# The last chunk's mix: one VectorE pass a tile, each tile on its own semaphore

## The reference, cut to what matters

```python
top2_w = np.exp(top2_l)
top2_w /= top2_w.sum(-1, keepdims=True) + 1e-09
out = np.zeros((N, D), dtype=np.float32)        # N = 2304 tokens, D = 512
for e in range(E):
    for k in range(2):
        mask = top2[:, k] == e
        h = np.maximum(x[mask] @ w1[e], 0.0)
        out[mask] += top2_w[mask, k, None] * (h @ w2[e])
```

## Time and profile before

| what | value |
|---|---|
| median of 3 runs | 1107.4 us (1107.07 to 1108.57) |
| the profiled execution's own time | 1106.87 us |
| its span, first to last instruction | 1105.0 us |
| granted TensorE clock, mean | 0.994 |
| PE busy | 1076.4 us (97%) |
| DVE / ACT / POOL busy | 52% / 29% / 36% |

### The profile page before, as it was taken

One profiled execution on the slowest core, in us unless ns is written; L12 is line 12 of the kernel. 1 busy time (PEld: TensorE's weight loads), 2 busy tenths in 40 slices (PEclk: granted clock), 3 DMA queues, 4 the chain that ended last, 5 costly groups with the idle time before them and its releaser, 6 DMA issues.

```text
span 1105.0 us, 20155 instructions
## 1 busy us (share of the span) xinstructions
PE 1076.4 (97%) x6113; PEld 939.6 (85%) x6114; DVE 575.4 (52%) x1209; ACT 324.3 (29%) x713; POOL 398.7 (36%) x370
## 2 busy tenths in 40 slices
PE   8999999999999999999999999999999999999994
PEld 7878999999998999999987788888888888888883
DVE  6776335254353353353447765565565565565461
ACT  7996123232331432432352102030303020200341
POOL 3557993022022022020185306070706051431485
PEclk9999999999999999999999999999999999999998
DMA  7975527013013012010084526271625253422675
GB/s 215 274 242 192 172 86 276 1 58 115 1 58 116 1 62 92 1 58 1 28 249 159 139 61 186 43 204 38 196 51 170 65 148 92 117 73 61 171 229 187
DMA packets 167356, 129.40 MB, mean 117 GB/s; under 512 B 96720, under 2 KB 128864, under 8 KB 167296
## 3 DMA queue, kind: packets, MB, share of 16 engines
q1 hardware_dynamic: 145440, 71.20, 22.9%
q10 hardware_dynamic: 16032, 38.47, 10.5%
q0 software_dynamic: 5824, 18.95, 5.1%
HBM read 85.87 MB, written 42.73 MB: 116 GB/s over the span
## 4 chain that ended last, share of the span: by engine, by line
PE 87%; POOL 3%; issue 3%; DMA 2%; ACT 2%; DVE 1%; another core or an unknown queue 0%; SPq 0%; POOLq 0%; ACTq 0%; DVEq 0%
PE bank L793 26%; PE bank L957 19%; PE bank L973 18%; PE bank L825 13%; PE bank L986 3%; PE bank L739 2%; PE bank L766 1%; POOL token_rows_a L680 1%; PE bank L749 1%; PE bank L733 1%; DMA token_rows_b<-expert_rows,slots_u 1%; PE bank L861 1%; ACT p_sb L1108 1%; POOL token_rows_a L693 1%; PE bank L872 1%
## 5 line engine op out<-in xcount | busy, mean ns | idle before, releaser
L793 PE MATMUL bank<-x_parts,mlp_weights 128*128 128x384 f32 x1704 | 312.0, 337 | 0.4 <-issue 0.3
L793 PEld LDWEIGHTS bank<-x_parts,mlp_weights 128*128 128x128 f32 x1704 | 296.8, 188 | 6.3 <-issue 1.2
L957 PE MATMUL bank<-expert_parts,xT_high 128*128 (+1 forms) x688 | 216.6, 396 | 1.5 <-DVE xT_low L1653 1.5
L973 PE MATMUL bank<-expert_parts,hT_high 128*128 (+1 forms) x688 | 213.3, 391 | 3.9 <-DVE hT_low L1664 3.9
L662 POOL TENSOR_TENSOR expert_parts<-raw_expert_a,expert_parts 128x512 fp32r<-128x512 f32 x64 | 81.4, 1304 | 240.6 <-ACT expert_parts L1255 240.4
L825 PE MATMUL bank<-mlp_weights,hidden_parts 128*128 128x512 f32 x648 | 162.2, 394 | 1.3 <-ACT y_sb L1179 1.3
L973 PEld LDWEIGHTS bank<-expert_parts,hT_high 128*128 128x128 f32 x688 | 129.7, 189 | 31.7 <-POOL expert_parts L662 2.8
L957 PEld LDWEIGHTS bank<-expert_parts,xT_high 128*128 128x128 f32 x688 | 125.6, 188 | 26.1 <-issue 2.2
L825 PEld LDWEIGHTS bank<-mlp_weights,hidden_parts 128*128 128x128 f32 x648 | 120.0, 188 | 25.1 <-ACT y_sb L1179 1.6
L973 PE MATMUL bank<-expert_parts,hT_low 128*128 (+1 forms) x344 | 134.6, 391 | 0.0
L957 PE MATMUL bank<-expert_parts,xT_low 128*128 (+1 forms) x344 | 134.3, 390 | 0.0
(11 more groups left out here) (206 smaller groups left out, 1225.1 us busy)
## 6 DMA issues: line engine op xcount, KB each, us to landing
raw_expert_a<-in_w ACTq DMA_DIRECT2D x32, 512.0 KB
raw_expert_b<-in_w ACTq DMA_DIRECT2D x32, 512.0 KB, 4.5
x_row<-routed_rows SPq DMA_DIRECT2D x172, 64.0 KB
expert_rows<-y_row SPq DMA_DIRECT2D x43, 256.0 KB
expert_rows<-zeros SPq DMA_DIRECT2D x4, 2304.0 KB, 12.6
v_sb<-in_v SPq DMA_DIRECT2D x32, 256.0 KB, 3.5
q_sb<-in_qT SPq DMA_DIRECT2D x16, 288.0 KB, 3.7
k_sb<-in_kT SPq DMA_DIRECT2D x16, 288.0 KB, 4.1
```

The source lines that it names most:

```text
L793: last = nc.tensor.matmul(bank[:, 0:CHUNK], w_sb[:, i, wp, at:at + P], xp[:, par, part, k, :], start=n == 0, stop=n == 3 * KB - 1)
L957: last = nc.tensor.matmul(ps[half][:, 0:512], (xTh, xTl)[xp][:, buf, k, :], ew_sb[:, bass.ds(slot, 1), wp, k * F2 + half * 512:k * F2 + ha ...
L973: last = nc.tensor.matmul(ps[5][:, 0:D], (hTh, hTl)[hp][:, f, :], ew_sb[:, bass.ds(slot, 1), 2 + wp, f * D:(f + 1) * D].rearrange("p a n - ...
```

## The change

For chunks 0 to 4 nothing changes. For chunk 5 the second rows are gathered on three semaphores, one a tile, in place of one; ACT no longer scales them and POOL no longer adds. In their place DVE, behind its last `y_row` copy, does one SCALAR_TENSOR_TENSOR a tile: second rows times their weight plus the first rows, which ACT has scaled as before. DVE waits for each tile's own gather, and counts `last_mixed`, for which ACT waits before each of the last three output DMAs.

```diff
-        second_in = [sem(f"second_in_{i}") for i in range(CHUNKS)]
+        second_in = [sem(f"second_in_{i}") for i in range(CHUNKS - 1)]
+        last_second_in = [sem(f"last_second_in_{t}") for t in range(CHUNK_TILES)]
+        last_mixed = sem("last_mixed")
...
-                gather_chunk(c, 1, second_in[c])
+                if c < CHUNKS - 1:
+                    gather_chunk(c, 1, second_in[c])
+                else:
+                    for t in range(CHUNK_TILES):
+                        gather(chunk_rows(c, 1)[:, t, :], slots_u[:, CHUNK_TILES * c + t, 1:2], last_second_in[t])
                 if c + 2 < CHUNKS:
                     gather_chunk(c + 2, 0, first_in[c + 2])
                 if 1 <= c < CHUNKS - 1:
                     add(c - 1)
-            add(CHUNKS - 1)
...
             for c in range(CHUNKS):
-                scale(c, 1, second_in, second_scaled)
+                if c < CHUNKS - 1:
+                    scale(c, 1, second_in, second_scaled)
                 if c + 2 < CHUNKS:
                     scale(c + 2, 0, first_in, first_scaled)
                 if c >= 1:
...
             for t in range(CHUNK_TILES):
-                act.wait_ge(rows_added, CHUNK_TILES * c + t + 1)
+                act.wait_ge(last_mixed, t + 1)
                 act.dma_start(out_rows(c)[:, t, :], chunk_rows(c, 1)[:, t, :]).then_inc(rows_out, 16)
...
             dve_hT(dve, t)
             dve_y(dve, t)
 
+
+            dve.wait_ge(first_scaled, CHUNK_TILES * CHUNKS)
+            for t in range(CHUNK_TILES):
+                dve.wait_ge(last_second_in[t], 16)
+                n, row = CHUNK_TILES * c + t, chunk_rows(c, 1)[:, t, :]
+                nc.vector.scalar_tensor_tensor(out=row, in0=row, scalar=kept[:, 1, n:n + 1],
+                                               in1=chunk_rows(c, 0)[:, t, :], op0=ALU.mult, op1=ALU.add
+                                               ).then_inc(last_mixed, 1)
```

## The result

The changed kernel takes 1100.33 us (median of 6 runs, 1098.47 to 1103.67), the kernel before 1107.24 us (6 runs, 1105.75 to 1108.57): a ratio of 0.994, 95% interval 0.9925 to 0.9955, 6.9 us less. The profiled execution took 1099.18 us with a span of 1097.3 us. POOL's stage and PE's also shift against each other: DVE's last copy starts 4.1 us after that issue before, 4.8 us after it here, and 3.9 to 5.1 us after it in the other profiles of these kernels. Where the end hangs on that copy, the distance from the copy's start is given too.

The account below looks back on a forecast made before the run. POOL's closing DRAIN, last at the barrier by 3.8 us, was taken to bound the end. Afterwards the outputs' branch, 1097.8, plus 0.2 gave span 1098.0, 7.0 us less: 1099.9 profiled, plus 0.5 for the median, 1100.4 us; range 1099.3 to 1104.9.

Parts of the forecast that it names:

- two branches: At the block's end, the later sets the span: POOL's last operation plus 6.09 us, or last tile mixed plus 2.03 plus 0.2.
- outputs' path: Third gather lands 1094.8, its mix ends 1095.55, outputs land 1097.6, SP at the barrier 1097.8: 3.2 us earlier than before.
- 6.09 us as a fixed length behind POOL's last operation: POOL's closing DRAIN ends 6.09 us after its last operation, now the third gather: 1091.45 + 6.09 = 1097.55; chance 0.42.
- A: Rival: POOL's closing DRAIN waits for the gathers to land, then takes 6.09 us: 1103.5 us; chance 0.30 together with A2.
- A2: Rival: POOL's closing DRAIN takes 8.64 us from where its row starts: 1102.7 us; chance 0.30 together with A.
- the sign: Length of POOL's closing DRAIN, beginning at about 1091.5: about 6.1 us for the forecast, 9.6 A, 8.6 A2, 13.4 C.
- out(4) at 1087.9, just behind the add of chunk 4: ACT issues chunk 4's 768 KB output at about 1087.9 in place of 1094.18, 6.3 us earlier, just ahead of the first gather.
- The third gather 4.29 us to landing, from the row of chunk 4: Chunk 5's third gather shares the DMA engines with out(4), landing after 4.29 us in place of 3.65, at 1094.8.
- turn-taking rule: A DMA engine alternates between queues packet by packet: third gather delayed 0.1 to 0.2 us, sum 0.5 us lower; not taken.
- Gathers one and two have time to spare: Chunk 5's first two gathers have 2.5 and 1.3 us of lead, so their mixes are over by the third's landing.
- The mix at 745 ns, one on the path: Each DVE mix of 128x512 takes 745 ns; only the last is on the path, from 1094.8 to 1095.55.
- Output 2.03 us to landing: The last output DMA lands 2.03 us after its issue, at 1097.6.

Follow-up runs that it names:

- half a DRAIN saved in the kernel before: Kernel before with one more DRAIN on POOL before the output stage's first gather: ratio 0.9977 to the kernel before, tail 14.1 us against 17.0.
- second profile: The changed kernel run and profiled once more, nothing altered: ratio 0.9938 to the kernel before, tail 10.1 us against 9.9.
- memset kernel: Changed kernel plus one 128x8 memset on POOL that waits for the three mixes: ratio 0.9982 to the kernel before, tail 14.0 us.
- the one with one wait: Changed kernel, but DVE waits for all three gathers of chunk 5 before its first mix: ratio 0.9955 to the kernel before, tail 11.7 us.
- the one on ACT and POOL: Kernel before with tile-by-tile waits and chunk 4's output DMA early, ACT still scaling and POOL adding: ratio 0.9991 to the kernel before, tail 16.1 us.

## Why the prediction was right

Right in sign and size, and in the mechanism of two branches. One step of the outputs' path did not happen: the last mixes wait for no gather. That the median, 1100.33 us, lies within 0.1 us of 1100.4 is luck, with six runs from 1098.47 to 1103.67. Step by step:

- *Two branches, POOL's the later one.* Shown: a memset on POOL alone gives back 4.1 of 7.1 us, and half a DRAIN saved in the kernel before gives 2.9 us.
- *6.09 us as a fixed length behind POOL's last operation.* It measured 6.1 us again. It was the open number, with 0.42 of the chance. A (6.09 from the gathers' landing on) and A2 (8.64 from the row's start) would have had POOL last; the DRAIN took 9.8 us from its row's start and was not last. A length counted from POOL's last operation came true; what makes it up, 82 ns a DMA, the forecast did not know. Its fit is partly luck, since 3.0 us behind the third gather's landing gives the same end in this kernel. And the sign was badly chosen: the forecast put 6.1 us for itself and 9.6 for A as the length of the row, from a start at 1091.5. The row began at 1087.2, so its 9.8 us would have been read as A; only the DRAIN's end less the end of POOL's last operation tells.
- *out(4) at 1087.9, just behind the add of chunk 4.* 1087.26, 0.03 us behind the add (1083.49 + 3.74 = 1087.23). POOL's stage was 0.6 us earlier in this execution, PE's was not: the last copy starts at 1092.18 against 1092.07. With the gathers earlier, the end hangs on the copy: 1092.79 + 2.07 + 2.03 + 0.4 = 1097.3, and not 1098.0.
- *The third gather 4.29 us to landing, from the row of chunk 4.* 4.1 us in the changed kernel, 4.3 in its second profile and in the memset kernel, 4.4 to 4.5 in the kernel that has only this move and in the one with one wait, 4.0 in the one on ACT and POOL. Against 3.65 that is 0.35 to 0.8 us of delay. The turn-taking rule of the Trainium skill, DMA: Bandwidth & Descriptors, section Queues, rings and completion order, was reckoned to give 0.1 to 0.2 us, so the row was the better guide.
- *Gathers one and two have time to spare.* Too easy: the first takes 4.9 to 5.1 us in every kernel with out(4) ahead of it, where no more than 4.3 were assumed. The trace of before had shown it, on the first gather of chunk 4, issued 0.12 us behind out(2):

```profile
L680 POOL DMA_INDIRECT token_rows_b<-expert_rows,slots_u x1: 969/969/969, 1076.4 to 1076.4; - x1
DMA to landing us min/median/max: 5.0/5.0/5.0
```

In the changed kernel it lands at 1092.5, 0.3 us before the first mix, because DVE is busy with the last expert tile's copy to 1092.87 anyway. In the memset kernel, where the copy lies 0.9 us earlier against the gathers, the first mix waits 0.58 us for it and the third 0.23 us for its own gather.
- *The mix at 745 ns, one on the path.* 746 ns at the median. The rule of the Trainium skill, VectorE: DVE Perf Modes, section on the TRN2 errata, stated there for a tensor_tensor, was 55 ns low at 691, as at the other size. But all three mixes are on the path, behind the copy, and overlap a little: 2.07 us from 1092.79. The forecast path, landing plus one mix, would end at 1094.0 + 0.75 = 1094.8, 0.1 us before that, so the error cost next to nothing.
- *Output 2.03 us to landing.* 2.0 us: 1094.87 to 1096.9.

The parts, as the profiles show them: the mix moved from ACT and POOL to DVE (the change against tile by tile on ACT and POOL) 6.2 us; of the change's own parts the wait tile by tile is worth 1.6 to 1.8 and the early out(4) 2.2 to 2.6 us when taken out of it, and out(4) -0.8 us when put in alone. They don't add up, since what counts is the later of two branches.

## What to carry to other kernels

Look at the block's end first: here the engine that came last to the barrier set the time. If that is POOL, with many DMAs of its own, take away its last compute operation or give it a DRAIN in an idle stretch before its final work. When two branches end within a few tenths of a microsecond, as here now, shortening either alone is worth nothing; the early DRAIN in the changed kernel shows it for POOL's branch. A DMA that is freed to start earlier meets whatever is issued next: price it for the first transfer behind it (here 1.8 us more), not only the last (0.35 to 0.8 us).

## What was not expected of the hardware

POOL's DRAIN costs 82 ns for every DMA of 128 rows that POOL has issued since its last DRAIN: 0.04, 0.13, 3.00 and 5.95 us with 0, 1, 36 and 72 gathers, with all of them landed 3 us and more before it; a DRAIN in between takes its share off the next (3.1 and 3.0 us in place of 6.1). The DRAINs of ACT and SP, which issue many DMAs too, take 0.15 and 0.01 us.
